# Attention into a gated MLP on one core: GpSimd splits all low halves of w_out, and the prologue and block 0 run in a new order

## The reference

```python
# q, k, v: (4, 8, 576, 64); w_in: (512, 2048); w_out: (2048, 512)
q_d, k_d, v_d = means of q, k, v over groups of 4 tokens
out_up = repeat(softmax(q_d k_d^T / 8) v_d, 4)                  # pooled attention
out_local = softmax(q k^T / 8 where |i - j| < 4, else -1e9) v   # band of 7 keys
x = (out_up + out_local) as (2304 tokens, 512)
h = x @ w_in
g = h * tanh(log(1 + exp(h)))                                   # mish
out = g @ w_out                                                 # (2304, 512)
```

## Time and profile before

| what | value |
|---|---|
| median of 3 runs | 510.17 us (505.64 to 510.19) |
| the profiled execution | 505.87 us, span 504.1 us |
| granted TensorE clock, mean | 0.995 of 2.4 GHz |
| TensorE busy | 487.2 us (97%) |
| VectorE, ScalarE, GpSimd busy | 219.1, 176.0, 121.2 us |
| read by DMA | 29.66 MB |

### The profile page before, as it was taken

The page is one execution under the profiler, slowest core; times in us unless marked ns, Lnnn a source line. Parts: engine busy times, 40 slices in busy tenths (PEclk is TensorE's granted clock), DMA queues, the critical chain, the costliest instruction groups (busy, mean ns, idle before and its releaser), DMA issues.

```text
span 504.1 us, 9597 instructions
## 1 busy us (share of the span) xinstructions
PE 487.2 (97%) x4040; PEld 434.7 (86%) x4040; DVE 219.1 (43%) x390; ACT 176.0 (35%) x399; POOL 121.2 (24%) x164
## 2 busy tenths in 40 slices
PE   7789999999999999899999989999999999999997
PEld 7678888988999988788898978989899998999996
DVE  5845875665322234536356363644222222232221
ACT  4664865462211123534353452534121111211111
POOL 3997546524100003134141322412000000000000
PEclk9989999999999999999999999999999999999999
DMA  8995522131200001503213051220010000100001
GB/s 283 334 315 160 203 74 59 48 106 34 89 1 0 1 2 47 169 1 106 59 48 105 3 168 37 70 59 1 1 62 1 0 1 0 44 21 1 0 2 62
DMA packets 15836, 35.01 MB, mean 69 GB/s; under 512 B 1840, under 2 KB 1968, under 8 KB 15792
## 3 DMA queue, kind: packets, MB, share of 16 engines
q1 hardware_dynamic: 15792, 34.38, 21.5%
HBM read 29.66 MB, written 4.72 MB: 68 GB/s over the span
## 4 chain that ended last, share of the span: by engine, by line
PE 86%; issue 3%; DVE 3%; ACT 3%; DMA 2%; POOL 2%; SPq 0%; ACTq 0%; POOLq 0%; DVEq 0%
PE acc L600 38%; PE hidden L583 36%; PE att L478 2%; PE att L491 2%; PE att L537 2%; PE att L507 1%; PE att L544 1%; PE att L519 1%; DMA k_t<-in_k 1%; DMA out<-stage 1%; POOL prob L381 1%; DMA v_win<-in_v_win 1%; POOL prob_pool L389 1%; DVE x_low L802 1%; PE hidden L537 1%
## 5 line engine op out<-in xcount | busy, mean ns | idle before, releaser
L814 DVE CAST g_high<-hidden 128x384 fp32r<-128x384 f32 x96 | 53.4, 557 | 205.3 <-PE acc L600 160.0
L583 PE MATMUL hidden<-x_high,w_in_high 128*128 128x384 f32 x384 | 130.2, 339 | 0.5 <-DVE g_low L816 0.5
L583 PE MATMUL hidden<-x_high,w_in_low 128*128 128x384 f32 x384 | 129.4, 337 | 0.0
L583 PE MATMUL hidden<-x_low,w_in_high 128*128 128x384 f32 x384 | 128.9, 336 | 0.0
L1006 ACT ACTIVATE hidden<-hidden 128x384 f32<-128x384 f32 x96 | 45.7, 476 | 234.2 <-PE hidden L583 233.9
L600 PE MATMUL acc<-w_out_high,g_high 128*128 128x512 f32 x288 | 115.0, 399 | 0.0
L600 PE MATMUL acc<-w_out_high,g_low 128*128 128x512 f32 x288 | 113.4, 394 | 0.0
L600 PE MATMUL acc<-w_out_low,g_high 128*128 128x512 f32 x288 | 113.3, 393 | 0.0
L583 PEld LDWEIGHTS hidden<-x_high,w_in_high 128*128 128x128 f32 x384 | 72.1, 188 | 4.8 <-DVE g_low L816 0.8
L583 PEld LDWEIGHTS hidden<-x_low,w_in_high 128*128 128x128 f32 x384 | 72.1, 188 | 3.1
L583 PEld LDWEIGHTS hidden<-x_high,w_in_low 128*128 128x128 f32 x384 | 72.0, 188 | 0.0
(11 more groups left out here) (93 smaller groups left out, 452.6 us busy)
## 6 DMA issues: line engine op xcount, KB each, us to landing
v_win<-in_v_win SPq DMA_DIRECT2D x16, 384.0 KB, 4.2
v_in<-in_v SPq DMA_DIRECT2D x16, 320.0 KB, 3.6
k_t<-in_k SPq DMA_DIRECT2D x16, 292.0 KB, 3.8
q_t<-in_q SPq DMA_DIRECT2D x16, 288.0 KB, 2.8
out<-stage SPq DMA_DIRECT2D x17, 256.0 KB, 2.1
w_in_raw<-in_w_in SPq DMA_DIRECT2D x16, 256.0 KB, 12.5
w_out_raw<-in_w_out SPq DMA_DIRECT2D x16, 256.0 KB, 5.0
out<-last_stage SPq DMA_DIRECT2D x1, 256.0 KB, 2.1
```

The source lines that it names most:

```text
L583: last = nc.tensor.matmul(hidden[:, g % HB, 0:TB], w, x[:, k, cols], start=(k == 0 and i == 0), stop=(k == KT - 1 and i == 2))
L814: nc.vector.tensor_copy(g_high[:, g % GB], x).then_inc(g_rounded, 1)
```

## The change

`low_out` moves from VectorE to GpSimd for all 16 tiles, with a semaphore of its own, `w_out_split_pool`, on which `second_product(0, f)` waits. All engines' lists for the prologue and block 0 are in a new order; they hold the same calls. SyncE gets waits on the landing of earlier loads between its loads, so that about four loads are under way, and its loads of v, q and k stand further ahead of w_in and w_out. The code after block 0 stays as it is. The diff, cut after the prologue on each engine:

```diff
@@ -53,6 +53,7 @@
 EARLY_IN = 5
 EARLY_OUT = 3
 ROUNDED_OUT = 2
+OUT_BY_POOL = (0,1,2,3,4,5,6,7,8,9,10,11,12,13,14,15,)
 
 EXP_TABLES = "natural_log_exp_and_others"
 MISH_TABLES = "mish"
@@ -227,6 +228,7 @@
         w_in_split = sem("w_in_split")
         w_out_rounded = sem("w_out_rounded")
         w_out_split = sem("w_out_split")
+        w_out_split_pool = sem("w_out_split_pool")
         hidden_ready = sem("hidden_ready")
         mish_ready = sem("mish_ready")
         g_rounded = sem("g_rounded")
@@ -284,27 +286,43 @@
                         sp.dma_start(out[TB * j + P * t:TB * j + P * (t + 1), :], staged(m)).then_inc(stored[m % 2], 16)
 
                 sp.dma_start(const[:], const_l).then_inc(const_loaded, 16)
+                load_qk(0)
                 load_w_in(0)
-                load_qk(0)
+                sp.wait_ge(qk_loaded[0], 32)
+                load_qk(1)
+                sp.wait_ge(w_in_loaded[0], 16)
+                load_qk(2)
+                sp.wait_ge(qk_loaded[1], 32)
+                load_qk(3)
+                sp.wait_ge(qk_loaded[2], 32)
+                load_v(0)
+                sp.wait_ge(qk_loaded[3], 32)
+                load_v(1)
+                sp.wait_ge(v_loaded[0], 32)
                 load_w_in(1)
+                sp.wait_ge(v_loaded[1], 32)
+                load_qk(4)
                 load_w_out(0)
-                load_qk(1)
-                load_qk(2)
+                sp.wait_ge(w_in_loaded[1], 16)
                 load_w_in(2)
-                load_v(0)
-                load_v(1)
-                load_qk(3)
+                sp.wait_ge(qk_loaded[0], 64)
                 load_w_in(3)
                 load_w_in(4)
-                load_qk(4)
+                sp.wait_ge(w_in_loaded[2], 16)
+                load_v(2)
+                sp.wait_ge(w_in_loaded[3], 16)
+                load_w_out(1)
+                sp.wait_ge(v_loaded[2], 32)
+                load_v(3)
+                sp.wait_ge(w_out_loaded[1], 16)
+                load_v(4)
+                sp.wait_ge(v_loaded[3], 32)
                 load_w_in(5)
-                load_w_out(1)
-                load_v(2)
+                load_w_in(6)
+                sp.wait_ge(v_loaded[0], 64)
                 load_w_out(2)
-                load_v(3)
-                load_v(4)
-                load_w_in(6)
                 for f in range(7, FT):
+                    sp.wait_ge(w_in_loaded[f - 3], 16)
                     load_w_in(f)
                 sp.wait_ge(out_ready, AHEAD)
                 for f in range(EARLY_OUT, 6):
@@ -395,55 +413,76 @@
                     nc.gpsimd.tensor_tensor(w_in_low[:, f], w_in_raw[:, f], w_in_high[:, f].bitcast(F32),
                                             ALU.subtract).then_inc(w_in_split, 1)
 
+                def low_out(f):
+                    pool.wait_ge(w_out_rounded, f + 1)
+                    nc.gpsimd.tensor_tensor(w_out_low[:, f], w_out_raw[:, f], w_out_high[:, f].bitcast(F32),
+                                            ALU.subtract).then_inc(w_out_split_pool, 1)
+
                 pool_q(0)
                 pool_q(1)
                 pool_q(2)
+                normalize_band(0)
                 normalize_pooled(0)
-                normalize_band(0)
                 pool_v(0)
+                pool_q(3)
                 normalize_band(1)
                 normalize_pooled(1)
-                pool_q(3)
+                pool_v(1)
                 normalize_band(2)
-                pool_v(1)
-                pool_q(4)
+                low_in(0)
                 normalize_pooled(2)
                 pool_v(2)
+                pool_q(4)
+                low_in(1)
                 normalize_band(3)
                 normalize_pooled(3)
-                low_in(0)
                 pool_v(3)
-                low_in(1)
-                pool_v(4)
                 low_in(2)
                 low_in(3)
                 low_in(4)
+                low_out(0)
                 low_in(5)
+                low_out(1)
                 low_in(6)
-                pool_q(5)
+                normalize_band(4)
+                low_out(2)
                 low_in(7)
-                normalize_band(4)
+                pool_v(4)
                 normalize_pooled(4)
                 low_in(8)
+                pool_q(5)
+                low_out(3)
+                low_out(4)
                 pool_v(5)
+                low_out(5)
+                low_in(9)
+                normalize_pooled(5)
+                low_in(10)
+                normalize_band(5)
+                low_in(11)
+                low_out(6)
+                low_out(7)
+                low_in(12)
                 pool_q(6)
-                normalize_band(5)
-                normalize_pooled(5)
-                low_in(9)
-                low_in(10)
-                low_in(11)
+                low_out(8)
+                normalize_pooled(6)
+                normalize_band(6)
                 pool_v(6)
-                low_in(12)
-                normalize_band(6)
-                normalize_pooled(6)
+                low_in(13)
+                low_out(9)
+                low_in(14)
+                low_out(10)
                 pool_q(7)
-                low_in(13)
-                low_in(14)
+                pool_v(7)
+                low_out(11)
+                low_out(12)
+                low_out(13)
+                normalize_band(7)
...
@@ -590,7 +629,11 @@
                     if g == 0:
                         pe.wait_ge(x_split, split(AHEAD - 1))
                     if j == 0:
-                        pe.wait_ge(w_out_split, f + 1)
+                        by_pool = sum(i <= f for i in OUT_BY_POOL)
+                        if f in OUT_BY_POOL:
+                            pe.wait_ge(w_out_split_pool, by_pool)
+                        else:
+                            pe.wait_ge(w_out_split, f + 1 - by_pool)
                     pe.wait_ge(g_split, g + 1)
                     for t in range(TT):
                         if f == 0 and j > 0:
@@ -606,18 +649,18 @@
 
                 keep_busy(WARM_UP)
                 keep_busy(BUSY)
+                band_scores(0)
+                pooled_scores(0)
                 keep_busy(BUSY)
-                band_scores(0)
+                band_scores(1)
                 keep_busy(BUSY)
-                pooled_scores(0)
-                busy_for_outputs(0)
-                band_scores(1)
+                keep_busy(BUSY)
                 pooled_scores(1)
+                turn_band(0)
                 band_scores(2)
-                keep_busy(BUSY)
-                turn_band(0)
                 turn_pooled(0)
                 pooled_scores(2)
+                busy_for_outputs(0)
                 outputs(0)
                 band_scores(3)
                 busy_for_turns(1)
@@ -628,25 +671,25 @@
                 outputs(1)
                 pooled_scores(3)
                 turn_band(2)
+                band_scores(AHEAD)
                 turn_pooled(2)
                 busy_for_outputs(2)
                 outputs(2)
-                band_scores(AHEAD)
                 busy_for_turns(3)
                 turn_band(3)
+                pooled_scores(AHEAD)
                 turn_pooled(3)
                 busy_for_outputs(3)
                 outputs(3)
                 first_product(0, 0, range(KT - 1))
                 first_product(0, 1, range(KT - 1))
                 first_product(0, 0, range(KT - 1, KT))
-                pooled_scores(AHEAD)
                 first_product(0, 1, range(KT - 1, KT))
+                second_product(0, 0)
                 first_product(0, 2)
                 first_product(0, 3)
-                second_product(0, 0)
+                turn_band(4)
                 first_product(0, 4)
-                turn_band(4)
                 turn_pooled(4)
                 second_product(0, 1)
                 outputs(4)
...
@@ -830,87 +873,71 @@
                 band_maxima(1)
                 pooled_inverses(0)
                 pooled_maxima(1)
+                pool_k(2)
+                band_maxima(2)
                 band_inverses(1)
-                pool_k(2)
+                band_inverses(2)
                 pooled_inverses(1)
-                band_maxima(2)
-                pooled_maxima(2)
-                band_inverses(2)
                 combine(0)
                 split_x(0)
+                pooled_maxima(2)
+                band_maxima(3)
                 pool_k(3)
-                band_maxima(3)
                 pooled_inverses(2)
                 combine(1)
                 band_inverses(3)
+                pool_k(4)
                 split_x(1)
                 pooled_maxima(3)
+                band_maxima(4)
                 pooled_inverses(3)
                 combine(2)
-                pool_k(4)
                 split_x(2)
-                low_out(0)
                 combine(3)
+                band_inverses(4)
                 split_x(3)
+                pooled_maxima(4)
```

(126 more changed lines are left out.)

34 lines of the change are left out of this document (8 added, 26 removed).

## The result

The changed kernel takes **516.76 us** (median of 4 runs, 515.51 to 516.96) against 508.84 us of the kernel before, run beside it (505.64 to 510.19): a ratio of **1.0156, 95% interval 1.0111 to 1.0201**. It is slower by 8 us. The profiled execution took 516.96 us with a span of 515.1 us, 11.0 us more than the span before.

What follows compares the result with a forecast made beforehand. TensorE's order was taken to fix the time, with time to win only in the prologue of about 50 us. 505.87 + 1.4 (late mish(0)) - 1.0 (holes) + 1.0 (clock) = 507.3 us; range 503.0 to 512.0.

Steps and rivals of the forecast that it cites:

- Part 3: SyncE's waits on landings: w_out(3) issued at 42.5 us, round_out(3) delays mish(0) to 46.5 instead of 45.10, +1.4 us.
- My bound of 3.5 us: Upper value for one w_in or w_out hop, issue to landing; 2.9 us was taken.
- rival B: Slower: eight serial hops 0.5 us longer each, mish(0) 5.4 us late, 512.0 us or 516 in the upper level; chance 0.13.
- The second consumer: pool_k(5) before split_g(1) on VectorE: pair 5's k lands at 48.5 us, hidden behind two products, costs nothing.
- Part 2: New order of the prologue, a serial relay over four pairs of heads: outputs(3) ends at 39.4 to 42 us, middle 40.5.
- the cover of 0.4 us: w_in(2), landed at 22.7 and rounded at 23.1 us before copy_band(1) on ScalarE; any loss beyond goes into outputs(1).
- Part 1: Sixteen low halves of w_out go from VectorE to GpSimd: nothing added, some 2 us of cover in the worst place.
- Part 4: Rest of block 0: no wait reaches TensorE after split_g(0), so three small holes go, -1.0 us.
- The clock: Half clock in useful products behind TensorE's idle time from 44.6 to 47.7 us: 0 to +1.7, taken +1.0 us.
- Rival A: SyncE keeps up, w_out(3) issued at outputs(3): 504.2 us, or 502.5 without "issue" holes in the relay; chance 0.26.
- The page's rule: If prologue "issue" holes are instruction fetches stuck in full DMA engines, fewer loads gain outputs(3) up to 3.0 us.
- The upper level: Runs of before at 510.2 us, read as a level 4.4 us higher; the changed kernel's median there near 511.

Runs made afterwards that it cites:

- run 1: Changed kernel with all 24 of SyncE's waits on landings taken out, order kept: 507.33 us, ratio 0.9982 against the kernel before.
- run 3: Changed kernel, all waits kept, only round_out(3) moved on ScalarE from before mish(0) to behind pooled_exp(4): 513.87 us, ratio 1.0122.
- run 6: Changed kernel, its order of loads, with waits placed so that eight loads may be under way instead of four: 507.28 us, ratio 0.9979.
- run 7: Kernel before, changed only by moving the sixteen low halves of w_out to GpSimd, in idle places of its old order: 507.64 us, ratio 0.9997.
- run 8: Changed kernel with 40 matmuls of zeros put in front of second_product(0,0), into the hole: 514.41 us, ratio 1.0146.
- run 9: Kernel before with WARM_UP = 6 instead of 10, 8 matmuls of zeros fewer at the start of TensorE's stream: 507.88 us, ratio 1.0009.
- run 10: Changed kernel without the 24 waits and with round_out(3) and pool_k(5) later: 506.64 us, ratio 0.9973.
- run 11: Changed kernel with eight loads under way instead of four, and round_out(3) and pool_k(5) later: 507.28 us, ratio 0.9998.
- run 4: Changed kernel, all waits kept, round_out(3) moved behind pooled_exp(4) and pool_k(5) behind split_g(3): 509.35 us, ratio 1.0032.

## Why the prediction was wrong

**The mechanism of Part 3 and its place were right, its size was wrong.** w_out(3) late on SyncE, round_out(3) idle on a DMA in front of mish(0), TensorE waiting on g_low after two products: all three are in the trace, and runs 1 and 3 show that they are the cause. The step that failed is the price of a hop. I took 2.9 us for w_in, near the lone load of 2.7, and 4.2 for v_win. Measured on the chain: v(0) 6.96 where I had 4.2, w_in 3.71 to 5.51 (2.70 once), v(2) 5.47. So w_out(3) was issued at 49.97, not 42.5, and itself took 4.95 us, not 3.3: +10.4 us for mish(0) instead of +1.4, which is 9.0 of the 9.6 us by which the measured change of the profiled execution (11.0) misses mine (1.4). Of the 7.5 us by which w_out(3) was issued later than forecast, 5.0 were lost by the landing of v(3) (37.02, not 32.0), 2.8 of them in v(0)'s hop alone, and 2.5 in the w_in hops behind it.

The medians of v and k came from quiet stretches with two loads under way. The 2.7 us are those of a load issued into an empty queue; the next one, issued 0.4 us behind it in the same trace of before, already took 4.1:

```profile
L278 SPq DMA_DIRECT2D w_out_raw<-in_w_out x1: 992/992/992, 41.6 to 41.6; - x1
...
DMA to landing us min/median/max: 4.1/4.1/4.1
```

The three loads of 256 KB issued 0.48 us apart at 48.1 to 49.0 took 4.9, 5.1 and 5.3 us, so they landed about 0.68 us apart. By these rows, as an estimate, some 2.0 of the 2.7 us of a load in an empty queue are not transfer: with more under way a load waits for those ahead, and at each hop of a chain of waits those 2.0 us come again. My bound of 3.5 us, and rival B's 0.5 us a hop, were both too near, although the row with 5.1 us stood beside them. No run parts the two ways of the theory, the lower rate and the hops: run 6 takes both away.

The Trainium skill (DMA: Bandwidth & Descriptors, "Anatomy of one DMA — SWDGE (gpsimd) path") gives a DMA that GpSimd issues a fixed part of about 2 us beside its bytes, most of it the confirmed write; the loads here are issued by SyncE, for which it has no such sum. The 2.7 us for 256 KB in an empty queue, less 0.68 for the transfer, agree with it all the same. Four loads under way can't hide that part, eight can: 227 to 232 GB/s in the six profiles with four, 295 in run 6 with eight.

**The second consumer.** Part 3 put pool_k(5) at nothing, hidden behind second_product(0,0) and first_product(0,2). In the changed kernel it was hidden behind the larger hole; run 3 shows it bare, 4.3 us.

**Part 2**: outputs(3) ended at 46.1 us, not 40.5. This did not count by itself, since TensorE had both first products done at 50.6 and stood still until 57.27. The relay was right as a relay; its inputs were late. v(0) landed at 18.64, not 15.5, and w_in(2) at 26.57, not 22.7: the cover of 0.4 us that I named was gone, and ScalarE stood 2.58 us in front of copy_band(1). The forecast had this as the sign of rival B, which was the right case (slower) but priced at 5.4 us for mish(0).

**Part 1** held: no wait on w_out_low, and run 7 is level. **Part 4** held: the holes of 1.03 us are gone (busy 84.97 of 84.97 us). Without the clock the same 768 matmuls also have 0.85 us less of busy time, which makes -1.9 instead of -1.0; where that comes from no row says.

**The clock**: +2.5 us instead of +1.0. The granted clock was at the lower level (1.2 GHz) behind the long hole, in products that count, and run 8, with the hole filled, has 1.00 there. An earlier fall (0.50 in 40:42, behind a hole of 2.12 us) slowed pair 3's transposes.

**Numbers in the working.** Three don't come out of their own rows; none is in the sum. From mish(0) at 46.5, with the 1.71 us of before from mish(0) to TensorE going on the earlier trace rows, split_g(0) would be through at 48.2, not 47.7. If hops of 3.5 us put w_out(3) at 45 and 2.9 at 42.5, then 2.7 puts it at 41.7, not 41. Rival A's 502.5 has no sum behind it: 504.2 less the holes' 3.0 would be 501.2.

**The page's rule** (instruction fetch) came true in what it gives, smaller holes with fewer loads under way, but won nothing: with four under way the two shrank from 3.0 to 0.25 us, and the waits cost 9.4 us. That fetching is the mechanism no run shows. The upper level near 510 us is no level: single runs of before lie anywhere from 505.15 to 510.78, and the profiles above put 3 us of such a spread into the prologue.

## What to carry to other kernels

Before putting waits between loads, work out the rate from loads under way and the time from issue to landing of *that* queue, not of a lone load; four of 256 to 384 KB gave 230 GB/s here, eight 295. A serial chain multiplies each error of a hop, so a hop's range belongs into the forecast times the number of hops. And when a queue gets slower, look for the consumer that now stands first: here two calls moved by a few places were worth most of the loss (7.4 of 9.4 us).

## What the runs showed of the hardware

TensorE has holes that belong to its instruction stream: in the seven profiles with full DMA engines (before, runs 1, 6, 7, 9, 10 and 11), whatever the order of work, they open behind the 344th or 345th and the 470th matmul, 0.4 to 3.5 us long (before 1.69 and 1.31; run 1 1.43 and 3.47; run 6 2.39 and 1.33); five of the seven have both, run 7 only the first and run 11 only the second. With four loads under way they are 0.25 us or not there. In run 10 there is a third, 0.29 us, another 125 matmuls on, behind the 595th:

```profile
41.32 0.43 PE L560 MATMUL acc<-prob_t,v_win 54*64 54x48 f32 x11 [0.29 <-issue]
```

So they come where the DMA engines are full (295 to 297 GB/s in the first 40 us, 290 in run 9); among those profiles nothing seen here orders their size. Behind a long one the granted clock is down (0.50 from 34 to 42 us in run 1). Other idle times put down to "issue" (up to 1.34 us, run 4) stand in front of a pair's outputs, where TensorE has waits, also with four under way; they are not meant here. The Trainium skill (Runtime: NRT & Kernel Launch, "Instruction fetch mechanics") has each engine fetch its instructions by DMA in blocks of 256 instructions; 125 matmuls with their weight loads between the two holes are 250 instructions, and the few others between them are not in these counts, which agrees. That the DMA fetch itself is late was not seen, only place and size.

Two engines' subtractions side by side cost both. With the sixteen low halves on VectorE each took 0.94 us in the mean against a median of 0.69, and GpSimd's other work took 4 us more than in run 7, where they are on GpSimd.
